# Feed-forward half of an attention kernel: three 512-token chunks of both batches in place of two 768-token batches in 384-column halves

## What is computed

```python
mask = q_bucket[:, :, :, None] == k_bucket[:, :, None, :]
scores = np.where(mask, scale * np.matmul(q, k.transpose(0, 1, 3, 2)), -1000000000.0)
attn_out = np.matmul(softmax(scores), v)
x = attn_out.transpose(0, 2, 1, 3).reshape(B * S, H * D)            # 1536 x 512
h = np.maximum(np.maximum(x @ w1, x @ w2), x @ w3)                  # 1536 x 768
x = h @ w_out                                                       # 1536 x 512
h = x @ w_in                                                        # 1536 x 2048
g = np.where(h > 0.0, h, np.exp(np.minimum(h, 0.0)) - 1.0)
return g @ w_out2
```

## Time and profile before

| | |
|---|---|
| time, median of 3 runs | 778.21 us |
| lowest and highest | 777.1 and 780.05 us |
| span of the profiled execution | 777.8 us |
| its own time | not listed apart from the span |
| TensorE busy in the span | 745.1 us, 96% |
| mean granted TensorE clock | 0.994 |
| DMA | 62.56 MB, mean 80 GB/s |

### The profile page before, as it was taken

How to read it: one execution, slowest core, us unless ns; L and a number is a source line. 1 busy time by engine, 2 the same in 40 slices (tenths; PEclk the granted TensorE clock), 3 DMA queues, 4 the chain that set the end, 5 groups by cost and what they waited for, 6 DMA issues and landing times.

```text
span 777.8 us, 11623 instructions
## 1 busy us (share of the span) xinstructions
PE 745.1 (96%) x3920; PEld 677.1 (87%) x3920; DVE 388.9 (50%) x616; ACT 396.5 (51%) x748; POOL 369.3 (47%) x294
## 2 busy tenths in 40 slices
PE   4699999989999998999999999999999999999997
PEld 3488888868888877999998998999999998998996
DVE  3677888877888874322214333333322214333333
ACT  1268879777887885222225444443322225444442
POOL 5177889877988997332123332331332123332330
PEclk9999999999999999999999999999999999999999
DMA  6756363562615300411122112122511122112112
GB/s 135 172 116 147 85 130 88 117 148 52 148 42 130 103 0 1 115 48 42 41 67 82 55 58 77 54 82 92 151 42 42 41 68 82 54 55 79 54 41 81
DMA packets 81515, 62.56 MB, mean 80 GB/s; under 512 B 28992, under 2 KB 72768, under 8 KB 81472
## 3 DMA queue, kind: packets, MB, share of 16 engines
q1 hardware_dynamic: 81472, 62.02, 30.6%
HBM read 38.81 MB, written 3.15 MB: 54 GB/s over the span
## 4 chain that ended last, share of the span: by engine, by line
PE 57%; ACT 1%; DVE 1%; DMA 0%; issue 0%; DVEq 0%
PE banks L677 14%; PE banks L679 14%; PE banks L678 13%; PE banks L1039 6%; PE banks L1040 6%; PE banks L1042 5%; DVE gl L973 0%; DVE g_sb L970 0%; DMA out_dram<-out_sb 0%; ACT neg L922 0%; ACT gh L924 0%; PE banks L1048 0%; ACT neg L920 0%; DVE out_sb L981 0%; ACT out_sb L931 0%
## 5 line engine op out<-in xcount | busy, mean ns | idle before, releaser
L868 POOL TENSOR_TENSOR wl<-raw,wh 128x1024 fp32r<-128x1024 f32 (+3 forms) x50 | 126.3, 2526 | 317.7 <-ACT wh L900 317.7
L331 POOL TENSOR_TENSOR p_lo<-probs,p_hi 128x384 fp32r<-128x384 f32 x192 | 200.1, 1061 | 64.8 <-ACT p_hi L379 63.9
L378 ACT ACTIVATE probs<-banks 128x384 f32<-128x384 f32 x192 | 94.9, 494 | 46.4 <-PE banks L606 44.0
L478 DVE TENSOR_REDUCE half_max<-banks 128x1 f32<-128x384 f32 x192 | 99.3, 547 | 34.3 <-PE banks L593 33.1
L677 PE MATMUL banks<-xh,wh 128*128 128x384 f32 x288 | 96.5, 335 | 0.4 <-PEq L126 0.3
L679 PE MATMUL banks<-xh,wl 128*128 128x384 f32 x288 | 96.2, 334 | 0.0
L678 PE MATMUL banks<-xl,wh 128*128 128x384 f32 x288 | 96.2, 334 | 0.0
L379 ACT ACTIVATE p_hi<-banks 128x384 fp32r<-128x384 f32 x192 | 94.4, 492 | 0.0
L964 DVE TENSOR_SCALAR g_sb<-banks 128x384 f32<-128x384 f32 x64 | 35.5, 557 | 116.6 <-ACT neg L920 116.6
L677 PE MATMUL banks<-yh,wh 128*128 128x384 f32 x256 | 86.0, 336 | 0.0
L679 PE MATMUL banks<-yh,wl 128*128 128x384 f32 x256 | 85.9, 336 | 0.0
(11 more groups left out here) (114 smaller groups left out, 1495.8 us busy)
## 6 DMA issues: line engine op xcount, KB each, us to landing
operands<-wh SPq DMA_DIRECT2D x36, 384.0 KB, 7.0
raw<-in_moe_w SPq DMA_DIRECT2D x36, 256.0 KB, 3.8
raw<-in_moe_w_in SPq DMA_DIRECT2D x32, 256.0 KB, 2.7
raw<-in_moe_w_out SPq DMA_DIRECT2D x32, 256.0 KB, 2.9
wl<-wh SPq DMA_DIRECT2D x12, 384.0 KB, 5.8
q_raw<-in_q SPq DMA_DIRECT2D x16, 192.0 KB, 3.5
k_raw<-in_k SPq DMA_DIRECT2D x16, 192.0 KB, 3.7
v_raw<-in_v SPq DMA_DIRECT2D x16, 192.0 KB, 2.4
```

The lines of the kernel that those rows point to most:

```text
L331: pool.tensor_tensor(p_lo[:, at, :], probs[:, step % RING, :], p_hi[:, at, :].bitcast(FP32), ALU.subtract).then_inc(pl_done, 1)
L378: act.activation(probs[:, step % RING, :], scores, ACT.Exp, scale=SCALE)
L478: dve.tensor_reduce(half_max[:, m % 2, n // 2, n % 2:n % 2 + 1], mx_ps[n % 2][:, 0:HALF], AX.X, ALU.max).then_inc(mx_read, 1)
L868: pool.tensor_tensor(wl[:, j, 0:cols], raw[:, j, 0:cols], wh[:, j, 0:cols].bitcast(FP32), ALU.subtract).then_inc(w_ready, 1)
```

## The change

Only the second half changes (and the five early products). The 1,536 tokens of both batches are taken as three chunks `c` of 512. Chunk 1 holds the last 256 tokens of batch 0 and the first 256 of batch 1, so its moving operand is a pattern of two pieces (`x_tokens`). `hh` and `hl` hold all 1,536 tokens; `yh` and `yl` take the place of `xh` and `xl`.

- All matmuls of the second half are now 512 columns wide. Experts: 18 units of 36 matmuls in two sets of three banks. Project: 12 of 18. `hidden`: 48 steps of 12, in four banks (4 to 7). `result`: 48 steps of 12, in banks 0 to 3. That is 1,440 of 512 columns in place of 1,920 of 384, and 576 in `result` as before.
- The expert and project weights are loaded and split once. The ff weights are loaded and split three times, `w_in` and `w_out2` of a tile by their own instructions (512 columns each) in place of one of 1,024.
- No loops: every engine's program is written out.
- The output copies and stores of a chunk are put into the next chunk's first steps.

```diff
+CHUNK = 512
+CHUNKS = B * S // CHUNK
+UNIT_ORDER = [(0, 0), (1, 0), (0, 1), (0, 2), (1, 1), (1, 2)] + [(m, c) for m in range(2, M1) for c in range(CHUNKS)]
+def x_tokens(x, t, c):
+    at = t * S + c * CHUNK
+    if c == 0:
+        return x[:, at:at + CHUNK]
+    if c == CHUNKS - 1:
+        at += (KD - 1) * S
+        return x[:, at:at + CHUNK]
+    whole, rest = x[:], CHUNKS * CHUNK // B - CHUNK
+    return bass.AP(whole.tensor, whole.offset + at, [whole.ap[0], [KD * S - CHUNK, 2], [1, rest]])
@@ EARLY, in the attention's block
-                    for c, x in EARLY:
-                        if (c, x) == (1, 0):
+                    for u, x in EARLY:
+                        if (u, x) == (1, 0):
+                            pe.wait_ge(w_ready, 2)
@@ feed_forward
-        yh = sb("yh", [P, KD * S], FP32R)
-        yl = sb("yl", [P, KD * S], FP32R)
+        yh = xh[:].rearrange("p (m n) -> p m n", m=KD)
+        yl = xl[:].rearrange("p (m n) -> p m n", m=KD)
-        acc = [banks[:, i, :] for i in range(T)]
-        two = banks[:, T:, :]
+        acc = [banks[:, i, :] for i in range(TILES_C)]
+        two = [banks[:, 2 * EXPERTS + i, :] for i in range(2)]
+        hid = [banks[:, TILES_C + i, :] for i in range(4)]
@@ sync, ff tiles
+            for n in range(STEPS_2):
+                if n > M2 and n % M2 == 4:
+                    store(n // M2 - 1)
+                sp.wait_ge(w_ready, W3_AT + n - 1 if n < 2 else in_count(n - 2))
+                sp.dma_start(raw[:, n % 2, 0:DM]..., w_in[...]).then_inc(in_loaded[n % 2], 16)
+                if n:
+                    load_out(n - 1)          # waits for out_count(n - 3)
@@ scalar
+            for n in range(STEPS_2):
+                act.wait_ge(s_ready, n + 1)
+                wait(act, g_done, n - 1)
+                act.activation(neg[:, n % 2, :], hid[n % 4], ACT.Relu, scale=-1.0).then_inc(relu_done, 1)
+                act.activation(neg[:, n % 2, :], neg[:, n % 2, :], ACT.Exp, scale=-1.0).then_inc(elu_exp, 1)
+                act.wait_ge(g_done, n + 1)
+                result_done(act, n - 2)
+                act.activation(gh[:, n % 2, :], g_sb[:, n % 2, :], ACT.Copy).then_inc(gh_done, 1)
+                if n and n % M2 == 0:
+                    store_half(n // M2 - 1)
+                if n + 2 < STEPS_2:
+                    ff_tile(n + 2)           # high part of in(n+2), after result(n-1), then of out(n+1)
@@ tensor
+            def hidden(n):
+                c = n // M2
+                pe.wait_ge(w_ready, in_count(n))
+                pe.wait_ge(yl_done, (KD - 1) * CHUNKS + c + 1)
+                wait(pe, pos_done, n - 3)
+                three(pe, hid[n % 4], [(weights(n % 2, t * P), moving(yh, yl, t, c)) for t in range(KD)]
+                      ).then_inc(s_ready, 1)
+            def result(n):
+                c, k = n // M2, n % M2
+                j, at = out_at(n)
+                pe.wait_ge(w_ready, out_count(n))
+                pe.wait_ge(gh_done, n + 1)
+                for t in range(TILES_C):
+                    if k == 0 and c:
+                        pe.wait_ge(out_copied[t % 2], (c - 1) * TILES_C // 2 + t // 2 + 1)
+                    pe.matmul(acc[t], gh[:, n % 2, cols], w2h, start=(k == 0), stop=False)
+                    pe.matmul(acc[t], gh[:, n % 2, cols], w2l, start=False, stop=False)
+                    if t == 0:
+                        pe.wait_ge(gl_done, n + 1)
+                    last = pe.matmul(acc[t], gl[:, n % 2, cols], w2h, start=False, stop=(k == M2 - 1))
+            hidden(0)
+            for n in range(STEPS_2):
+                if n + 1 < STEPS_2:
+                    hidden(n + 1)
+                result(n)
```

More of the change, by code:

```diff
@@ L735, in feed_forward @@
         elu_exp = sem("elu_exp")
-        pos_done = [sem(f"pos_done{c}") for c in range(2)]
+        pos_done = sem("pos_done")
         g_done = sem("g_done")
@@ L802, in first_of, with in_count @@
[L802 to L825, removed]
+        def in_count(n):
+            return W3_AT + 1 if n == 0 else W3_AT + 2 * n
@@ L827, in _, with out_count, out_at, result_done @@
+        def out_count(n):
+            return W3_AT + 2 * n + 3 if n < STEPS_2 - 1 else W3_AT + 2 * n + 2
+        def out_at(n):
+            return ((n + 1) % 2, DM) if n < STEPS_2 - 1 else (n % 2, 2 * DM)
+        def result_done(eng, n):
+            if n >= 0 and n % M2 == M2 - 1:
+                eng.wait_ge(out_ready, (n // M2 + 1) * TILES_C)
+            elif n >= 0:
+                eng.wait_ge(r_done, n + 1 - n // M2)
         @block.sync
         def _(sp):
[L829 to L859, removed]
+            def load_out(n):
+                j, at = out_at(n)
+                loaded = out_loaded[j] if n < STEPS_2 - 1 else out_loaded[2]
+                if n == 0:
+                    sp.wait_ge(w_ready, W3_AT)
+                elif n == 1:
+                    sp.wait_ge(w_ready, in_count(0))
+                elif n < STEPS_2 - 1:
+                    sp.wait_ge(w_ready, out_count(n - 2))
+                k = n % M2
+                sp.dma_start(raw[:, j, at:at + DM], w_out2[k * P:(k + 1) * P, :]).then_inc(loaded, 16)
@@ L861, in _ @@
+            load_out(STEPS_2 - 1)
+            store(CHUNKS - 1)
+            sp.wait_ge(stored, CHUNKS * TILES_C * 16)
         @block.gpsimd
         def _(pool):
[L863 to L869, removed]
@@ L927, in end, with split_hi, experts_tile @@
-            def end(b):
-                for t in range(0, T, 2):
-                    act.wait_ge(out_ready, b * T + t + 1)
-                    wait(act, stored, b * T * 16)
-                    act.activation(o_sb[:, t, :], acc[t], ACT.Copy).then_inc(out_copied[0], 1)
-            batches(act, work, split_hi, end)
+            def split_hi(j, at, cols):
+                act.activation(wh[:, j, at:at + cols], raw[:, j, at:at + cols], ACT.Copy).then_inc(w_split, 1)
+            def experts_tile(m):
+                act.wait_ge(w_loaded[m % 2], 48 * (m // 2 + 1))
+                act.wait_ge(f_ready, EXPERTS * UNITS_OF[m - 2])
+                split_hi(m % 2, 0, EXPERTS * DM)
@@ L935, in _ @@
+            store_half(CHUNKS - 1)
         @block.vector
         def _(dve):
[L937 to L975 removed]
@@ L977, in end, with store_half @@
-            def end(b):
-                for t in range(1, T, 2):
-                    dve.wait_ge(out_ready, b * T + t + 1)
-                    wait(dve, stored, b * T * 16)
-                    dve.tensor_copy(o_sb[:, t, :], acc[t]).then_inc(out_copied[1], 1)
-            batches(dve, work, end=end)
+            def store_half(c):
+                for t in range(1, TILES_C, 2):
+                    dve.wait_ge(out_ready, c * TILES_C + t + 1)
+                    wait(dve, stored, c * TILES_C * 16)
+                    dve.tensor_copy(o_sb[:, t, :], acc[t]).then_inc(out_copied[1], 1)
@@ L1017, in hidden, with moving @@
-            def hidden(b, k, j):
-                for c in range(2):
-                    if isinstance(k, int) and k == 0:
-                        pe.wait_ge(yl_done[c], (b + 1) * KD)
-                    else:
-                        pe.wait_ge(pos_done[c], k + b * M2)
-                    last = three(pe, two[:, c, 0:HALF],
-                                 [(weights(j, t * P), moving(yh, yl, t * S + c * HALF)) for t in range(KD)])
-                    last.then_inc(s_ready, 1)
-            def result(b, k, j, at):
-                first, final = isinstance(k, int) and k == 0, is_last(k)
-                pe.wait_ge(gh_done, k + (b * M2 + 1))
-                if not final:
-                    pe.wait_ge(gl_done, k + (b * M2 + 1))
-                g = k % 2 if isinstance(k, int) else 1 - j
+            def moving(h, l, t, c):
+                cols = slice(c * CHUNK, (c + 1) * CHUNK)
+                return h[:, t, cols], l[:, t, cols]
@@ new lines, in _ @@
+            for u, (m, c) in enumerate(UNIT_ORDER):
+                pe.wait_ge(w_ready, m + 1)
+                wait(pe, max_done, u - 1)
+                for x in range(EXPERTS):
+                    if (u, x) not in EARLY:
+                        expert(pe, banks, wh, wl, xh, xl, u, x, f_ready)
+            for v in range(KD * CHUNKS):
+                m, c = v // CHUNKS, v % CHUNKS
+                pe.wait_ge(w_ready, W2_AT + m + 1)
+                wait(pe, yl_done, v - 1)
+                pairs = [(weights(m % 2, t * P), moving(hh, hl, t, c)) for t in range(M1)]
+                pe.wait_ge(hl_done, UNIT_AT[M1 - 2, c] + 1)
+                three(pe, two[v % 2], pairs[:-1], stop=False)
+                pe.wait_ge(hl_done, UNIT_AT[M1 - 1, c] + 1)
+                three(pe, two[v % 2], pairs[-1:], start=False).then_inc(y_ready, 1)
@@ L1050, in result @@
-                if not final:
-                    last.then_inc(r_done, 1)
-            def work(b, kind, k, j):
-                pe.wait_ge(w_ready, k + (first_of(b, kind) + 1))
-                if kind == "experts":
-                    experts(b, k, j)
```

(9 more changed lines are left out.)

331 lines of the change are left out of this document (148 added, 183 removed).

## The result

The changed kernel takes 768.12 us (median of 4 runs, 767.84 to 768.18) against 777.66 us for the kernel before (4 runs on record by now, 777.1 to 780.05). The ratio is 0.9871, with a 95% interval from 0.9853 to 0.989: 1.3% faster. The forecast was 772.6 us with a range from 769.5 to 778.0. The profiled execution took 768.09 us and spans 766.3.

The account below looks back on a forecast made before the run. TensorE's own issue was taken to bound the second half: matmuls 456.8, barrier 0.5, steps 2.9, end waits 1.0, slow matmuls 0.5 make 461.7 us against 467.34, 5.6 less. Forecast 772.6 us, range 769.5 to 778.0.

Parts of the forecast that it names:

- The two rates and the matmul term: Second half: 0.1734 us per 384-column and 0.2267 per 512-column matmul; 480 fewer instructions save 6.5 us.
- Two-piece operand: Chunk 1's 216 matmuls reading two runs of 256 columns: taken at nothing, at most 2.9 us.
- early products: Start of the second half: the second unit's tile 1 is ready before TensorE gets there, so no wait.
- seams: Passages between batches, chunks and stages: the waits between batches go (0.26 and 0.39 us); chunk changes cost nothing.
- The chain behind hidden: ScalarE and VectorE work from hidden to gh and gl: only the first and last result wait, 0.5 us each.
- Steps of ff: Feed-forward: 48 steps with 0.06 us of disturbance each, 2.9 us, where before it was 1.8.
- the barrier: A TensorE wait in the second half, listed with the early products, said to remain at 0.5 us.
- Rival 5: Second half: the ff disturbance and the two end waits vanish, giving 768.7 us; chance 0.04.
- Rival 1: Wide matmuls cost by the column, all at the disturbed 0.2311 us, giving 778.9 us; chance 0.20.
- rival 2: Fixed cost of only 2.5 ns per matmul, so the saving is 1.2 us and the time 777.7; chance 0.03.
- 3 (late loads): Ff weight loads of 7.5 us arrive late, costing 12 us over the steps, giving 784.6 us; chance 0.07.
- 4 (loops): Loops did cost: 13 passes at 0.33 us on TensorE's sequencer, 4.3 us more saved, giving 768.3; chance 0.03.

Follow-up runs that it names:

- chunk384: The changed kernel with four chunks of 384 tokens in place of three of 512, so ff has 64 steps: 779.6 us, ratio 1.002 to the kernel before.
- unrolled: The kernel before with its feed-forward and expert-tile loops written out, nothing else: 779.69 us, ratio 1.0005 to the kernel before.
- two_banks: The changed kernel with hidden in two banks in place of four: 769.56 us.
- hidden384: The changed kernel with each hidden product streaming only 384 of its 512 columns, the rest left out: 741.44 us, one run.
- all384: The kernel before with result, from its second tile on, streaming 384 of 512 output columns, the rest left out: 748.59 us, one run.
- widths: The changed kernel with project (from its third product) streaming 320 and hidden 256 of 512 columns, the rest left out: 707.25 us, one run.

## Why the prediction was right in sign and short in size

**The two rates and the matmul term (6.5 us).** Right. By the finer starts, 1,920 x 0.1733 + 575 x 0.2267 = 463.1 against 2,015 x 0.2267 = 456.7: 6.4 us, and chunk384 takes it back. The fixed part of 13.3 ns holds at 256, 320, 384 and 512 columns. The Trainium skill's 2.5 ns for each matmul ("TensorE: Matmul & The Clock Gate", section "Back-to-back issue gap") does not fit these pairs of weight load and matmul. The prediction passed over that the section gives this figure for an isolated matmul; for a stream of such pairs it has about 131 ns at 512 columns, which this kernel, at 226.7, does not bear out either.

**Two-piece operand, loops, banks, weights split once, early products, seams.** All taken at nothing, and the runs show no cost of them, but for 0.13 us where project passes to ff: the undisturbed distances from 320 to 400 us include units of chunk 1, and unrolled and two_banks show theirs. Between the first and the last `result` no distance in the 48 steps shows a wait.

**The chain behind hidden.** Right at both ends: forecast 1.0 us, measured 0.5 at the first `result` and 0.6 at the last, with the slow matmuls behind, for which the forecast had 0.5 more. All waits of the forecast together, the barrier included, are 2.0 us; 2.2 were measured.

**Steps of ff, the term that failed.** "I keep 0.06 us of disturbance per step, as each has its own loads, splits and Relu: 2.9 us" was wrong. The disturbance is not of the neighbours but of the change from 384 to 512 columns and back, 0.067 us a step: hidden384 brings it back and all384 takes it away. In the changed kernel everything streams 512, so 30 x 0.067 = 2.0 us went, where I had 1.1 added: the term is 0 us and not 2.9. That is 2.9 of the 4.5 us by which the forecast missed; the term's lower bound was 1.8, not nothing. Rival 5, in which it vanishes, came near the time (768.7) with a chance of only 0.04, but in part by luck: its other half, that the two end waits vanish, did not come true, and terms at the end that it did not have made up for them. The evidence was there: in experts loads and splits run beside the matmuls too, and no distance is disturbed. Rival 1 argues just so, against the disturbance spreading; the step's term was not put to the same test.

**Left out: the end.** I costed what comes behind the last matmul at no change. The six tiles' backlog in the DMA queue is gone, and the span ends 3.6 us behind the last matmul, not 4.4: 0.8 us. Fewer tiles would give no more: chunk384 stores three at the end and also ends 3.6 us behind. Between the span and the run's time lie 1.8 us in all kernels of the changed form and 2.1 in those of the old (unrolled too): 0.35 us, whose cause stays open. Also wrong was to place the profile 0.4 us below the median, as if its span were its time: a time is its span and 2.1 us, so the profiled execution took near 780 and lies above the median. As the saving was taken off the median, this did no harm beyond 0.5 us of the median's own shift, from 778.21 to 777.66.

**The sum.** 6.4 (fewer matmuls) + 2.0 (one width) = 8.4 in the second half, with the other waits 2.2 us before and after; 0.8 at the end, 0.35 around the span: 9.5 us, as 777.66 - 768.12 is. That the two agree to 0.1 us is chance, since the interval of the ratio is 1.4 us wide to either side. From the forecast: 2.8 in the second half, 0.8, 0.35 and 0.55 make 4.5.

**Rivals.** Rival 1 (cost by the column) and 2 (2.5 ns) are refuted by the distances, 3 (late loads) by the waits, with loads landing in 2.7 us at 101 GB/s, 4 (loops) by unrolled; that its 768.3 is next to the measured time is chance. A slip in rival 2: the other terms add 0.9 us and not 0.7 (4.9 against 4.0), so its time is 777.9.

## What to carry to other kernels

Where TensorE is never idle, take the cost of a matmul from start-to-start distances at two widths and split it into columns and a fixed part; here 13.3 ns for each instruction made the step from 384 to 512 columns worth 0.8% of the kernel. One width throughout gave 2.0 us more and the shorter end 0.8; the rest of a large rebuild (weights split once, no loops, four banks) was worth nothing. A small excess that recurs at the same place of each step should be explained before it is carried over by count: look for a stage with the same neighbours and without it. Cost the end as well: here six tiles of 256 KB stored together kept the DMA engines full until 3.6 us behind the last matmul, while four or three landed 2.8 us behind it.

## What the hardware showed unexpectedly

A change of the streamed width between stretches of matmuls can cost time without a wait: about 0.03 us over the six matmuls after 512 to 384 columns, 0.04 over the nine after 384 to 512, alike in before, chunk384 and hidden384, and nothing in the one-width steps of all384 or of the changed kernel. From 512 to 256 or 320 columns, in widths, it costs nothing. Why is open. It looks like the tail of a stall: in the kernel before, behind the stall at 552.32 us in the earlier trace rows, where all matmuls are 384 columns wide, the distances rise in the same way, two of those shown to 0.18 us, before they are back at 0.173. That is an observation, not a cause.

```profile
552.75 0.41 PE L677 MATMUL banks<-xh,wh 128*128 128x384 f32 x1
553.00 0.34 PE L678 MATMUL banks<-xl,wh 128*128 128x384 f32 x1
...
553.53 0.35 PE L678 MATMUL banks<-xl,wh 128*128 128x384 f32 x1
553.71 0.34 PE L679 MATMUL banks<-xh,wl 128*128 128x384 f32 x1
553.89 0.34 PE L677 MATMUL banks<-xh,wh 128*128 128x384 f32 x1
```
